# Attention and two mixtures of experts on one core: scores from split q and k

## What is computed

```python
scores = scale * np.matmul(q, k.transpose(0, 1, 3, 2))
thresh = np.max(scores, axis=-1, keepdims=True) - tau
scores = np.where(scores >= thresh, scores, -1000000000.0)
attn = np.exp(scores - np.max(scores, axis=-1, keepdims=True))
attn = attn / (np.sum(attn, axis=-1, keepdims=True) + 1e-09)
x = np.matmul(attn, v)                      # then 2304 tokens x 512
e_idx = np.argmax(x @ w_gate + modality_bias[modality_id], axis=1)
x = gate_w * (np.maximum(x @ w1[e_idx], 0) @ w2[e_idx])   # per token, 8 experts, width 1024
h = x @ w_in                                # width 2048
out = (h * np.tanh(log1p(exp(min(h, 20))))) @ w_out
```

## Time and profile before

| | us |
|---|---|
| median of 3 runs (1013.97 to 1015.04) | 1014.14 |
| the profiled execution | 1012.94 |
| its span, first to last instruction | 1011.3 |

### The profile page before, as it was taken

One profiled execution on the slowest core, in us unless ns is written; L12 is line 12 of the kernel. 1 busy time (PEld: TensorE's weight loads), 2 busy tenths in 40 slices (PEclk: granted clock), 3 DMA queues, 4 the chain that ended last, 5 costly groups with the idle time before them and its releaser, 6 DMA issues.

```text
span 1011.3 us, 17645 instructions
## 1 busy us (share of the span) xinstructions
PE 969.3 (96%) x6176; PEld 805.7 (80%) x6177; DVE 675.2 (67%) x1223; ACT 505.0 (50%) x971; POOL 483.7 (48%) x573
## 2 busy tenths in 40 slices
PE   6999999999998999999999889999999999999995
PEld 4777777777777777888887678988989889899884
DVE  5788788888874641111114389879878788798783
ACT  4666666666664242222235355555555545555542
POOL 4222226766231176200000066777777777777874
PEclk9999999999999999999999999999999999999998
DMA  3112227222211456211114400001001000000000
GB/s 105 65 51 69 72 83 287 75 83 87 74 57 43 160 172 232 74 47 47 47 44 198 123 16 8 25 32 32 1 32 32 2 32 1 32 1 1 32 1 31
DMA packets 20440, 65.84 MB, mean 65 GB/s; under 512 B 3344, under 2 KB 3344, under 8 KB 19600
## 3 DMA queue, kind: packets, MB, share of 16 engines
q1 hardware_dynamic: 13040, 40.68, 11.7%
q0 software_dynamic: 4480, 18.42, 5.1%
q10 hardware_dynamic: 2848, 5.80, 2.0%
HBM read 46.63 MB, written 18.27 MB: 64 GB/s over the span
## 4 chain that ended last, share of the span: by engine, by line
PE 84%; DVE 6%; issue 3%; ACT 2%; DMA 2%; POOL 1%; ACTq 0%; DVEq 0%; POOLq 0%
PE psum L416 6%; PE psum L1280 6%; PE psum L1265 6%; PE psum L1263 6%; PE psum L1282 6%; PE psum L1281 6%; PE psum L1264 6%; PE psum L373 4%; PE psum L388 4%; DVE rr L1354 3%; PE psum L992 3%; PE psum L994 3%; PE psum L993 3%; PE psum L965 3%; PE psum L967 3%; PE psum L966 3%
## 5 line engine op out<-in xcount | busy, mean ns | idle before, releaser
L1354 DVE RECIPROCAL rr<-rr 128x384 f32<-128x384 f32 x96 | 244.1, 2542 | 0.9 <-ACT rr L1308 0.9
L1216 POOL TENSOR_TENSOR uu<-uu,ex 128x384 f32<-128x384 f32 x96 | 97.4, 1015 | 244.7 <-ACT uu L1302 244.6
L497 ACT ACTIVATE prob<-ssb,smin 128x576 f32<-128x576 f32 x144 | 111.6, 776 | 104.5 <-DVE ssb L600 103.2
L600 DVE TENSOR_SCALAR_CACHE_REDUCE ssb<-psum,tauk 128x576 f32<-128x576 f32 x144 | 112.6, 815 | 46.6 <-PE psum L376 37.6
L1263 PE MATMUL psum<-x2T_hi,w_in_hi 128*128 128x384 f32 x384 | 131.4, 342 | 5.3 <-DVE gg L1360 3.7
L1265 PE MATMUL psum<-x2T_hi,w_in_lo 128*128 128x384 f32 x384 | 130.0, 339 | 0.0
L1264 PE MATMUL psum<-x2T_lo,w_in_hi 128*128 128x384 f32 x384 | 129.4, 337 | 0.0
L294 POOL TENSOR_TENSOR limit<-smin,margin 128x2 f32<-128x2 f32 (+1 forms) x80 | 57.7, 722 | 147.4 <-DVE ssb L600 147.0
L1044 DVE TENSOR_TENSOR hT_lo<-psum,hT_hi 128x512 fp32r<-128x512 f32 x38 | 26.3, 691 | 149.1 <-ACT hT_hi L1021 149.1
L1280 PE MATMUL psum<-w_hi,g_hi 128*128 128x512 f32 x288 | 114.8, 398 | 4.3 <-ACT osb L1331 2.5
L1282 PE MATMUL psum<-w_hi,g_lo 128*128 128x512 f32 x288 | 113.8, 395 | 0.0
(11 more groups left out here) (205 smaller groups left out, 2214.8 us busy)
## 6 DMA issues: line engine op xcount, KB each, us to landing
qk<-in_qk_dram SPq DMA_DIRECT2D x16, 640.0 KB, 4.4
vsb<-in_v_dram SPq DMA_DIRECT2D x16, 512.0 KB, 3.4
xrow<-xs ACTq DMA_DIRECT2D x17, 288.0 KB, 2.8
ys<-ysb SPq DMA_DIRECT2D x19, 257.0 KB, 3.0
stage<-in_w_in_dram POOLq DMA_DIRECT2D x16, 256.0 KB, 3.3
wa<-in_wa_dram SPq DMA_DIRECT2D x2, 2048.0 KB, 8.3
wb<-in_wb_dram SPq DMA_DIRECT2D x2, 2048.0 KB, 13.6
yrow<-ys SPq DMA_DIRECT2D x5, 771.0 KB, 4.6
```

The costliest lines, as they stand in the source:

```text
L497: act.activation(prob[:, n % 3, cols], ssb[:, w, cols], ACT.Exp, bias=smin[:, w, h:h + 1], scale=-1.0).then_inc(exp_done, 1)
L600: dve.tensor_scalar(ssb[:, w, h * S:(h + 1) * S].rearrange("p (a q) -> p a q", a=2), b_bank if h else a_bank, factor, BIG, ALU.mult, ALU.m ...
L1354: dve.reciprocal(rr[:, n % 4], rr[:, n % 4]).then_inc(r_done, 1)
```

## The change

The scores of pairs 1 to 15 are made from split operands. q and k of a pair come from memory twice, stacked over the partitions: rows 0 to 63 and rows 64 to 127 hold the same head column by column, both heads beside each other in the free dimension.

- GpSimd casts q to fp32r for all 128 partitions (`q_high`, 1280 columns, step tt = 1 of the pair before), then overwrites half of the partitions of each head with q less its high part (`q_low`, two operations of 64 partitions and 640 columns, tt = 2), so a query tile stands over the array's rows as high part and low part. `k_low` (two operations of 64 partitions and 576 columns, tt = 3) makes the low part of k, one head in each half of the partitions.
- ScalarE casts k to fp32r (`k_high`, 1152 columns, after `evacuate` at tt = 2) and makes the block-diagonal high part of q for the rest tile (two copies of 64 partitions and 128 columns).
- TensorE: a full tile takes four fp32r matmuls of 128 rows by 288 keys, (high and low q) by high k, and four of 64 rows, high q by low k. The rest tile takes four of the first and two of 128 rows. Low by low is left out, as in the experts. `scores` of a pair's first tile waits for `q_low_done`, `q_rest_done` and `k_low_done`. Pair 0 keeps fp32 matmuls, with buffers and loads of its own.
- `limit`'s and `rsum`'s order on GpSimd stays; before an operation that follows a partial one GpSimd waits for its completion (`follows`). Scatters, weight loads, and the 32 pieces of the weights' split stand at new steps; the high and low operations of a piece are no longer neighbours.
- SyncE loads q and k separately, each into one buffer, after `q_low_done`, `q_rest_done`, and `k_low_done` of the pair before. From pair 12 on the buffers lie over `wa`.

The diff's core (left out: declarations, the host layout, part of the placing of buffers, waits of `scatter`):

```diff
@@ -48,11 +48,14 @@
 VCOLS = VTURN + QT * D
 ROUTE, RANK = PER + 3, 7
 EARLY = 3
-SCATTER_AT = RANK + 3
-LOAD_AT = ROUTE + RANK + 8
-CLEAR_AT = (ROUTE + RANK + 4) // TT + 2
 PIECES = WCOLS // 512
-SPLIT_AT = [c for c in range(LOAD_AT + 4, NS) if not SCATTER_AT <= (c - ROUTE) % PER <= SCATTER_AT + TT][:2 * PIECES]
+SCATTER_AT = [[35, 35, 39, 39, 40], [54, 54, 55, 55, 59], [74, 74, 75, 75, 76]]
+LOAD_AT = 34
+W1_HI_AT, W1_LO_AT = [40, 44, 44, 45, 45, 49, 49, 51], [41, 44, 45, 46, 49, 50, 50, 51]
+W2_HI_AT, W2_LO_AT = [56, 59, 59, 60, 60, 60, 61, 64], [64, 65, 65, 66, 69, 69, 70, 70]
+MOVED = 12
+QW = S + REM
+CLEAR_AT = 8
 ALL_CONSTS = 17
 GATE_COL, ID_COL = 0, 1
 YW = DM + 2
...
@@ -205,32 +218,43 @@
     OUT0 = 512 - 4 * HW
     row_bank = psum[:, 7, OUT0:512]
 
-    def q_of(u):
-        return qk[:, u, 0:S]
-
-    def k_of(u):
-        return qk[:, u, S:2 * S]
+    def q_raw_of(p):
+        return q_raw[p >= MOVED]
+
+    def k_hi_of(p):
+        return k_hi[p >= MOVED][p % 2]
 
     def sync(sp):
         sp.dma_start(taub[:], io["tau"].partition_broadcast(P)).then_inc(tau_in, 16)
-        for u in range(2):
-            sp.dma_start(qk[:, u], io["qk"][u]).then_inc(qk_in[u], 16)
-            sp.dma_start(vsb[:, u], io["v"][u]).then_inc(v_in[u], 16)
+        for h in range(2):
+            rows = slice(h * D, h * D + D)
+            sp.dma_start(q_first[rows, :], io["q_first"][rows, :]).then_inc(first_in, 16)
+            sp.dma_start(k_first[rows, :], io["k"][0, rows, h]).then_inc(first_in, 16)
+        sp.dma_start(vsb[:, 0], io["v"][0]).then_inc(v_in[0], 16)
         sp.dma_start(wg[:], io["w_gate"]).then_inc(small_in, 16)
         sp.dma_start(mb[:].rearrange("p m e -> p (m e)"),
                      io["mbias"].partition_broadcast(P)).then_inc(small_in, 16)
         sp.dma_start(modi[:].rearrange("p t c -> p (t c)"), io["mod"]).then_inc(small_in, 16)
-        for n in range(2, PAIRS):
+        for n in range(1, PAIRS):
             u = n % 2
             if n == CLEAR_AT:
                 sp.wait_ge(lead_ready, 1)
                 for i in range(EARLY):
                     row = sp.value_load(tab["early"][0:1, i:i + 1], min_val=i * P, max_val=(E - 1) * CAP + i * P)
                     sp.dma_start(io["xs"][bass.ds(row, P), :], t["zrow"][:]).then_inc(cleared, 16)
-            sp.wait_ge(scores_done, TT * (n - 1))
-            sp.dma_start(qk[:, u], io["qk"][n]).then_inc(qk_in[u], 16)
-            sp.wait_ge(pv_done, TT * (n - 1))
+            if n == MOVED:
+                sp.wait_ge(w1_ready, WP)
+            if n >= 2:
+                sp.wait_ge(q_low_done, 2 * (n - 1))
+                sp.wait_ge(q_rest_done, 2 * (n - 1))
+            sp.dma_start(q_raw_of(n)[:], io["q"][n]).then_inc(q_in, 16)
+            if n >= 2:
+                sp.wait_ge(k_low_done, 2 * (n - 1))
+            sp.dma_start(k_raw[:], io["k"][n]).then_inc(k_in, 16)
+            if n >= 2:
+                sp.wait_ge(pv_done, TT * (n - 1))
             sp.dma_start(vsb[:, u], io["v"][n]).then_inc(v_in[u], 16)
+        sp.wait_ge(scores_done, TT * (PAIRS - 1))
         sp.sem_inc(y_stored, 16 * YRING)
         sp.wait_ge(cleared, 16 * EARLY)
         sp.wait_ge(scattered, 16 * TT * (B - 1))
...
                 pool.tensor_copy(wx[rows, i, h, gate], wg[rows, i, :]).then_inc(wx_done, 1)
 
+        last, lows = [consts, ALL_CONSTS, False], [0]
+
+        def follows(signal, value, part=False):
+
+            if part or last[2]:
+                pool.wait_ge(last[0], last[1])
+            last[:] = [signal, value, part]
+
         def find_limit(n):
 
+            follows(limited, n + 1)
             w, k = n % 2, 2 if n % TT < QT else 1
             pool.wait_ge(copied, units(n + 1))
             if n >= 2:
...
@@ -322,16 +358,53 @@
             pool.dma_start(w_raw[:], io["wa"][bass.ds(lead, 1)]).then_inc(w1_in, 16)
             pool.dma_start(t["wb"][:], io["wb"][bass.ds(lead, 1)]).then_inc(w2_in, 16)
 
-        def split_lead(raw, landed, hi, lo, ready, piece, before):
+        def w_high(raw, landed, hi, own, piece):
 
             cols = slice(piece * 512, piece * 512 + 512)
             if piece == 0:
                 pool.wait_ge(landed, 16)
-            pool.tensor_copy(hi[:, cols], raw[:, cols]).then_inc(split_own, 1)
-            pool.wait_ge(split_own, before + piece + 1)
+            follows(own, piece + 1)
+            pool.tensor_copy(hi[:, cols], raw[:, cols]).then_inc(own, 1)
+
+        def w_low(raw, hi, lo, own, ready, piece):
+            cols = slice(piece * 512, piece * 512 + 512)
+            signal, value = (ready, piece // 2 + 1) if piece % 2 else (low_own, lows[0] + 1)
+            lows[0] += 1 - piece % 2
+            follows(signal, value)
+            pool.wait_ge(own, piece + 1)
             low = pool.tensor_tensor(lo[:, cols], raw[:, cols], hi[:, cols].bitcast(F32), ALU.subtract)
-            if piece % 2:
-                low.then_inc(ready, 1)
+            low.then_inc(signal, 1)
+
+        def q_high(p):
+
+            pool.wait_ge(q_in, 16 * p)
+            if p >= 2:
+                pool.wait_ge(scores_done, TT * (p - 1))
+            follows(q_hi_done, p)
+            pool.tensor_copy(q_split[p % 2][:], q_raw_of(p)[:]).then_inc(q_hi_done, 1)
+
+        def q_low(p):
+
+            pool.wait_ge(q_hi_done, p)
+            moved = sum(c < TT * (p - 1) + 2 for at in SCATTER_AT for c in at)
+            if moved:
+                pool.wait_ge(scattered, 16 * moved)
+            for h in range(2):
+                rows = slice((1 - h) * D, (2 - h) * D)
+                follows(q_low_done, 2 * p - 1 + h, True)
+                part = q_split[p % 2][rows, h]
+                pool.tensor_tensor(part, q_raw_of(p)[rows, h], part.bitcast(F32), ALU.subtract).then_inc(q_low_done, 1)
+
+        def k_low(p):
+
+            pool.wait_ge(k_hi_done, p)
+            if p >= 2:
+                pool.wait_ge(scores_done, TT * (p - 1))
+            for h in range(2):
+                rows = slice(h * D, (h + 1) * D)
+                follows(k_low_done, 2 * p - 1 + h, True)
+                pool.tensor_tensor(k_lo[p % 2][rows, :], k_raw[rows, h], k_hi_of(p)[rows, h].bitcast(F32),
+                                   ALU.subtract).then_inc(k_low_done, 1)
 
         pool.wait_ge(wx_done, 4 * HP)
         pool.wait_ge(coef_done, 1)
@@ -340,18 +413,33 @@
                 find_limit(c)
             if c >= 1:
                 add_eps(c - 1)
-            b, k = divmod(c - ROUTE, PER)
-            k -= SCATTER_AT if b else SCATTER_AT + 4
-            if b >= 0 and 0 <= k < TT:
-                scatter(b, k)
+            p, tt = c // TT + 1, c % TT
+            if p < PAIRS:
+                if tt == 1:
+                    q_high(p)
+                elif tt == 2:
+                    q_low(p)
+                elif tt == 3:
+                    k_low(p)
+            for b in range(B - 1):
+                for j in range(TT):
+                    if SCATTER_AT[b][j] == c:
+                        scatter(b, j)
             if c == LOAD_AT:
                 load_lead()
-            if c in SPLIT_AT:
-                piece = SPLIT_AT.index(c)
-                if piece < PIECES:
-                    split_lead(w_raw, w1_in, w1_hi, w1_lo, w1_ready, piece, 0)
-                else:
-                    split_lead(t["wb"], w2_in, w2_hi, w2_lo, t["w2_ready"], piece - PIECES, PIECES)
+            if c == W2_HI_AT[0]:
+                pool.wait_ge(scores_done, TT)
+            if c == W2_LO_AT[0]:
+                pool.wait_ge(scores_done, TT * MOVED)
+            for i in range(PIECES):
+                if W1_HI_AT[i] == c:
+                    w_high(w_raw, w1_in, w1_hi, split_own, i)
+                if W1_LO_AT[i] == c:
+                    w_low(w_raw, w1_hi, w1_lo, split_own, w1_ready, i)
+                if W2_HI_AT[i] == c:
+                    w_high(t["wb"], w2_in, w2_hi, w2_own, i)
+                if W2_LO_AT[i] == c:
+                    w_low(t["wb"], w2_hi, w2_lo, w2_own, t["w2_ready"], i)
         for tt in range(TT):
             scatter(B - 1, tt)
 
...
@@ -361,23 +449,47 @@
         def scores(n):
             p, tt = divmod(n, TT)
             u = p % 2
-            if tt == 0:
-                pe.wait_ge(qk_in[u], 16 * (p // 2 + 1))
             if n >= 1:
                 pe.wait_ge(copied, units(n))
-            q, k = q_of(u), k_of(u)
-            if tt < QT:
-                cols = slice(tt * P, (tt + 1) * P)
-                qa, qb = q[0:D, cols], q[D:P, cols]
-                ka, kb = k[0:D], k[D:P]
-                pe.matmul(a_bank[:, 0, :], qa, ka[:, 0:HALF], start=True, stop=True)
-                pe.matmul(b_bank[:, 0, :], qb, kb[:, 0:HALF], start=True, stop=True)
-                pe.matmul(a_bank[:, 1, :], qa, ka[:, HALF:S], start=True, stop=True)
-                pe.matmul(b_bank[:, 1, :], qb, kb[:, HALF:S], start=True, stop=True).then_inc(scores_done, 1)
-            else:
-                qr = qk[:, u, 2 * S:]
```

(69 more changed lines are left out.)

36 lines of the change are left out of this document (24 added, 12 removed).

## The result

The kernel after took 1056.89 us (1052.72 to 1057.28), the kernel before 1014.06 us (1013.04 to 1015.04): a ratio of 1.041 (95% interval 1.0385 to 1.0441), 43 us slower. The forecast was 1026, its range ended at 1037. The direction was right; the size forecast, 12 us, was under a third of what came. The profiled execution of after took 1052.72 us, with a span of 1051.0 against 1011.3.

A forecast was written before the change was run, and what follows sets the result against it. TensorE was taken as the bound, busy 96%. Pairs 1 to 14 +9.2, pair 0 +1.0, pair 15 -0.9, weight pieces +3: +12.3 on 1012.94, 1025.2; median 1026, range 1007 to 1037.

The forecast's parts named there:

- the lock: Port pair shared by GpSimd and VectorE: exclusive for the whole instruction against a VectorE operation with two SBUF inputs.
- both holdings: In each pair `q_low` holds VectorE's first `prob` at tt = 3 (5.21 to 6.45), `k_low` the rest tile's (8.78 to 9.14).
- the wait of TensorE: Before a pair's first scores TensorE idles some 1 us, released by `k_lo`.
- Rival 2: Lock hardly acts, on half the partitions or through interleaving; `k_low` in time: -8.4 us, 1006 (1003 to 1011); chance 0.23.
- rival 3: One of the two holdings disappears, pairs keep their old period but for some 0.05 us: 1014 to 1016; chance 0.10.
- rival 5: On TensorE half-height fp32r matmuls don't pair, or the switch is paid twice: +9 to +12, 1036 us; chance 0.05.
- rival 4: A waiting `k_low` yields to both `prob` operations: 0.74 us more for each of 15 pairs, 1037 us; chance 0.12.
- Scatters move by some steps, hidden: Scatters at new steps around attention: claimed to be hidden, with no time added to the sum.
- so nothing waits: SP's queue: q and k loads go out over 10 us before use, v as before; no wait counted.
- The term of the scores: TensorE's scores: 0.98 us for 1.16 in a full tile, 0.78 for 0.96 in the rest tile, 0.18 gained each.
- The worked pair: One pair timed from S (VectorE's score-copy start) of tt = 2: next pair's S at 12.45 for 11.39; +0.66 taken.
- The pieces: 32 pieces of the lead expert's weights moved to steps 40 to 70: +3 us for all, bounds 0 and 6.

The follow-up runs named there:

- E4: Kernel before with GpSimd's four 64-partition subtractions added in pairs 0 to 6, into a buffer nobody reads: 1013.84 us.
- E9: Kernel after with the subtractions of q and k cut to 8 columns, and their casts too in pairs 1 to 11: 1037.57 us, routing differs.
- E11: Kernel after with both weight loads issued at step 38 instead of 34, still on GpSimd's queue, first split pieces a few steps later: 1049.01 us.
- E12: Kernel after with the first weight load at step 38 and the second at step 43, on GpSimd's queue: 1042.51 us.
- E10: Kernel before with only the new steps for scatters, weight loads and weight pieces: 1017.06 us, ratio 1.0039.
- E3: Kernel after with the subtractions of `q_low` and `k_low` cut to 8 columns: 1026.25 us, routing differs; pairs 1, 3 and 4 about 18.5 us.
- E1: Kernel after with the two 2 MB weight loads on ScalarE's queue instead of GpSimd's, same step: 1046.15 us, ratio 1.0329.

## Why the prediction was right and wrong

**Right: the lock, both holdings, the wait of TensorE.** `prob` of 1.76 and 1.95 us at the two tiles, TensorE waiting for `k_lo`, `q_low` of 1.60 a half (forecast 1.53), and a held operation that resumes some 0.2 us before the recorded end of what holds it. Rival 2, that the lock hardly acts on half the partitions, falls with E4; rival 3 with pairs of 19.7 and more; rival 5's time with E9, where a pair without splitting is shorter than before, though its first ground came true (below); and of rival 4 the opposite is seen: both halves of `k_low` went through before the rest tile's masks.

**The step that failed: "Scatters move by some steps, hidden" and "so nothing waits".** 14.3 of the 30.7 us missing (43.0 found, 12.3 forecast) are in pair 7, and this is why: I went through SP's queue for q, k and v, and not through GpSimd's own, where the 4 MB now stand ahead of rows that a new instruction waits for. The wait was in the diff, at the head of `q_low`. E11 moved it to another pair (pair 7 was 12.7 us shorter), E12 took it away: 14.4 us of the whole by the medians, 13 by the ratios. It isn't the whole miss: E12's 1042.5 is still outside the range. E10 shows that the new order alone costs pair 7 nothing; it takes the two together.

**The term of the scores was mis-sized: 0.39 a pair for 0.9.** By steps, E9's pair 4, without splitting, took 3.66, 3.39, 4.13, 3.64 and 3.62 us, before's 3.84, 3.57, 3.94, 3.63 and 3.85: TensorE's 0.18 or more came in three of the five, nothing at tt = 3, and tt = 2 got 0.19 longer. In after, from 94.61 to 98.01 VectorE has work without a gap, so 3.39 us is its own length; the next step, 4.13 for the 3.72 that I took, begins with `pv` waiting 0.28 us for VectorE's `x`. I had written that VectorE waits for TensorE "by 0.30 us at tt = 3 and not at all at tt = 2", and yet let TensorE's gain through in full. What the five steps don't give is 0.5 a pair, about 8 us.

That TensorE's gain came to 0.18 a tile was luck: two errors cancelled. The six slots take 1.18 us (93.32 to 94.50), not 0.98, no less than before's four (106.43 to 107.61). Narrow windows part the two groups of four matmuls shown above (each row begins with the first matmul that hasn't ended yet):

```profile
93.55 0.56 PE L469 MATMUL psum<-k_hi0a,q_split 128*128 128x288 f32 x3
93.68 0.43 PE L469 MATMUL psum<-k_hi0a,q_split 128*128 128x288 f32 x2
93.81 0.29 PE L469 MATMUL psum<-k_hi0a,q_split 128*128 128x288 f32 x1
94.04 0.53 PE L478 MATMUL psum<-k_lo,q_split 64*128 64x288 f32 x4
94.28 0.30 PE L478 MATMUL psum<-k_lo,q_split 64*128 64x288 f32 x2
```

The stacked matmuls start 0.23, 0.13 and 0.13 apart, so the 0.13 was right, and my 0.20 for switching came as 0.10 behind the first and 0.09 ahead of the half-height ones. But the two slots of half-height matmuls take 0.24 and 0.22, where I had 0.13 each: as long as a slot of half-height fp32 passes before (0.24). That is the first ground of rival 5, "half-height fp32r matmuls don't pair", and 0.20 of the 0.26 us that its bound (-0.08 for 0.18) had put on it. Two of them start together, but together take nearly twice what one full-array matmul takes; whether they share the time or follow each other the trace doesn't tell. The weight loads don't set the spacing: each stacked matmul has its own, 0.189 us in the mean, longer than the 0.13:

```profile
L469 PEld LDWEIGHTS psum<-k_hi1a,q_split 128*128 128x128 f32 x60 | 8.6, 189 | 1.2 <-issue 1.0
```

The gain lies ahead of the scores, and I hadn't counted it there: from the start of `rows_out`'s two row matmuls to the first score there are 0.15 us (93.17 to 93.32) for 0.34 before (106.09 to 106.43), here of after and then of before:

```profile
93.17 0.41 PE L555 MATMUL psum<-wx,otsb 128*128 128x144 f32 x2
```

```profile
106.09 0.41 PE L443 MATMUL psum<-wx,otsb 128*128 128x144 f32 x2
106.43 0.51 PE L373 MATMUL psum<-qk 64*128 64x288 f32 x1
```

So after a wait nothing is gained, and from the start of the scores to S are 1.29 us (93.32 to 94.61), not the 1.11 of my sum.

**The worked pair: the mechanism held, its last link changed.** GpSimd was earlier than I had it: `k_low` ended at S + 10.86 (108.87 less 98.01), forecast 11.28. I had VectorE ask for the next mask during the first half, and get it between the two. It asked at 107.54, when the second half, 1.40 us before the end, had begun at 107.47. Instead VectorE came late: one mask held to 109.49, then the other, the normalising, the routing, and S at 110.87, that is 12.86 for 12.45. TensorE's scores had been there since 110.31 (109.02 + 1.29). So pairs 1, 3 and 4 lost 0.9 to 1.2 over before, for +0.66 forecast, and the holding costs 1.2 to 1.5 against E3 (in pair 3 0.3 of it comes and goes: it took 19.73 and 19.70 in E1 and E11).

**Not costed: the routing work.** I worked one pair and multiplied by 14. Pair 2 lost 1.7, pair 5 1.8 and pair 6 2.5 us, since there VectorE and GpSimd have other work and the casts, nearly free elsewhere, cost 1.1, 0.9 and 0.8 (E3 less E9). Pairs 0 to 6 got +10.7 for 5.0 forecast.

**The pieces: right alone, not in company.** E10 gives 2.9 us in pairs 8 to 14 for the +3 forecast. But pairs 8 to 14 lost 16.7: with short subtractions and the pieces (E3) 4.6 of them, with full subtractions 12.1 more, 1.7 a pair. How these split between pieces that GpSimd does beside a held VectorE and the routing wasn't taken apart further; in pair 8 some 1.3 us are TensorE's clock after the stall (step 4.99 for 3.67).

**Right but small:** ScalarE's split has cover (0.05 a pair with q's cast, E3 less E9; 0.3 was the bound). Pair 15, forecast -0.9, took +0.2.

**The range** missed for the same reason as the sum: all five cases were about one ordinary pair, and none was about a queue that the new instruction waits for, or about pairs with routing work.

## What to carry to other kernels

When an instruction gets a new wait on DMAs, list what stands ahead of those DMAs in their own queue, in the new order; 4 MB there cost 10.8 us of wait, and issuing the two loads later and apart took 14 us off. A subtraction on GpSimd that reads two tiles holds VectorE's two-input operations for nearly its whole length: awaited by nobody the four of a pair cost 0.2 us, on the path 1.2 to 1.5. Work out the pairs that have other work apart from the ordinary ones. A gain on the engine that bounds a pipeline is worth only the slack of the next one: here 0.39 of 0.9 us.

## What the runs showed of the hardware

GpSimd's hold on VectorE acts with 64 partitions too (a mask of 0.81 us took 1.76 and 1.95), and reaches small one-input operations (20 columns: 1.36 us for 0.17); a fill of 64 partitions didn't hold at all (0.82). Full-array fp32r matmuls of 288 columns start 0.13 us apart, though each loads its weights in 0.189; two half-height ones take 0.22 to 0.24 together, no less than two half-height fp32 passes (0.24). Rows scattered behind a load on GpSimd's queue moved no packet until nearly all of the load's had begun (11.7 us after the issue behind 4 MB, 7.4 behind 2 MB, 4.6 with the 4 MB on another queue, 2.3 with none). After a stall of 10.9 us TensorE's granted clock was at half, and the same four matmuls took 1.30 us for 0.77.
